# Attention in a fused attention and two-layer MLP kernel: full-row transposes of q and k, and another order of the steps of a pair

## The reference

```python
def _attn_ref(q, k, v, tau):            # q, k, v: 4 x 8 x 576 x 64
    scores = np.matmul(q, k.transpose(0, 1, 3, 2)) / np.sqrt(64)
    thresh = np.max(scores, axis=-1, keepdims=True) - tau
    scores = np.where(scores >= thresh, scores, -1e9)
    attn = np.exp(scores - np.max(scores, axis=-1, keepdims=True))
    attn = attn / (np.sum(attn, axis=-1, keepdims=True) + 1e-09)
    return np.matmul(attn, v)
# heads are put side by side: x is 2304 x 512
h = x @ w_in1; g = s * relu(h)**2 + b; x = g @ w_out1     # 512 -> 2048 -> 512
h = x @ w_in2; g = relu(h) + alpha * min(h, 0); out = g @ w_out2
```

## Time and profile before

| what | value |
|---|---|
| median of 3 runs | 1110.75 us (1110.47 to 1111.75) |
| the profiled execution | 1110.12 us, its span 1108.3 us |
| mean granted TensorE clock | 0.995 |
| busy: PE, DVE, ACT, POOL | 1095.1, 525.2, 509.3, 257.9 us |

### The profile page before, as it was taken

How to read it: one execution, slowest core, us unless ns; L and a number is a source line. 1 busy time by engine, 2 the same in 40 slices (tenths; PEclk the granted TensorE clock), 3 DMA queues, 4 the chain that set the end, 5 groups by cost and what they waited for, 6 DMA issues and landing times.

```text
span 1108.3 us, 18964 instructions
## 1 busy us (share of the span) xinstructions
PE 1095.1 (99%) x5826; PEld 892.5 (81%) x5826; DVE 525.2 (47%) x1014; ACT 509.3 (46%) x946; POOL 257.9 (23%) x438
## 2 busy tenths in 40 slices
PE   7999999999999999999999999999999999999998
PEld 6777777777678888888888889888888888888897
DVE  5988888898633242242242236522322332332232
ACT  3878778787744332232232234544433333333343
POOL 2656666565564300000000004422000000000000
PEclk8999999999999999999999999999999999999999
DMA  8666565665111100000000003211100000010010
GB/s 194 144 148 155 136 154 141 148 148 129 44 51 48 54 1 1 1 0 0 0 0 0 0 8 89 86 48 38 39 0 0 30 8 0 0 38 0 0 39 20
DMA packets 86554, 59.28 MB, mean 53 GB/s; under 512 B 49376, under 2 KB 69872, under 8 KB 86512
## 3 DMA queue, kind: packets, MB, share of 16 engines
q1 hardware_dynamic: 82048, 57.28, 20.2%
q10 hardware_dynamic: 4464, 1.48, 0.6%
HBM read 30.94 MB, written 4.72 MB: 32 GB/s over the span
## 4 chain that ended last, share of the span: by engine, by line
PE 94%; DVE 3%; ACT 1%; issue 1%; DMA 0%; POOL 0%; ACTq 0%; POOLq 0%; DVEq 0%
PE psum L934 23%; PE psum L936 23%; PE psum L935 23%; PE psum L1068 6%; PE psum L1034 5%; PE psum L963 3%; PE psum L965 3%; PE psum L1063 2%; DVE act_r L870 2%; PE psum L944 2%; PE psum L1042 1%; ACT win_hi L589 1%; PE psum L1031 1%; PE psum L1073 1%; ACT act_r L704 0%
## 5 line engine op out<-in xcount | busy, mean ns | idle before, releaser
L936 PE MATMUL psum<-x_hi,win_lo 128*128 128x512 f32 (+1 forms) x640 | 238.7, 373 | 0.0
L934 PE MATMUL psum<-x_hi,win_hi 128*128 128x512 f32 (+1 forms) x640 | 238.2, 372 | 0.0
L935 PE MATMUL psum<-x_lo,win_hi 128*128 128x512 f32 (+1 forms) x640 | 238.2, 372 | 0.0
L935 PEld LDWEIGHTS psum<-x_lo,win_hi 128*128 128x128 f32 x640 | 120.2, 188 | 24.0
L934 PEld LDWEIGHTS psum<-x_hi,win_hi 128*128 128x128 f32 x640 | 120.3, 188 | 23.0
L936 PEld LDWEIGHTS psum<-x_hi,win_lo 128*128 128x128 f32 x640 | 120.2, 188 | 23.0
L881 DVE SCALAR_TENSOR_TENSOR act_r<-act_n,nalpha,act_r 128x512 f32<-128x512 f32 (+1 forms) x80 | 56.2, 702 | 160.1 <-ACT act_r L715 159.8
L870 DVE SCALAR_TENSOR_TENSOR act_r<-act_r,s_c 128x512 f32<-128x512 f32 (+1 forms) x80 | 72.4, 905 | 116.4 <-ACT act_r L704 116.4
L612 ACT ACTIVATE ex<-psum,negm 128x576 f32<-128x576 f32 x144 | 107.6, 747 | 39.9 <-DVE negm L786 38.8
L707 ACT ACTIVATE g_hi<-act_r,b_c 128x512 fp32r<-128x512 f32 (+1 forms) x80 | 54.5, 682 | 152.5 <-PE psum L936 122.4
L546 POOL TENSOR_SCALAR ex<-ex,none_in,rinv 128x576 f32<-128x576 f32 x142 | 117.5, 827 | 19.8 <-DVE rinv L805 13.4
(11 more groups left out here) (97 smaller groups left out, 1622.4 us busy)
## 6 DMA issues: line engine op xcount, KB each, us to landing
k_twice<-k_hi SPq DMA_DIRECT2D x64, 144.0 KB, 2.5
stage<-in_moe_w_out_dram SPq DMA_DIRECT2D x32, 256.0 KB, 2.5
out_dram<-stage SPq DMA_DIRECT2D x18, 256.0 KB, 2.2
q_both<-q_hi SPq DMA_DIRECT2D x32, 128.0 KB, 2.3
q_both<-q_lo SPq DMA_DIRECT2D x32, 128.0 KB, 2.3
win_raw<-in_moe_w_in_dram SPq DMA_DIRECT2D x16, 256.0 KB, 2.9
stage<-in_moe_w_in_dram SPq DMA_DIRECT2D x16, 256.0 KB, 2.6
raw_q<-in_q_dram SPq DMA_DIRECT2D x30, 128.0 KB, 2.4
```

The source lines that it names most:

```text
L934: nc.tensor.matmul(dst, lhs[0], rhs[0], start=first, stop=False)
L935: nc.tensor.matmul(dst, lhs[0], rhs[1], start=False, stop=False)
L936: return nc.tensor.matmul(dst, lhs[1], rhs[0], start=False, stop=final)
```

## The change

It does these things:

- `fill_qk` transposes the last 64 rows of q and k as full transposes of 128 rows; the rows 64 to 127 of that part of `raw_q` and `raw_k` are set to zero once by DVE. q takes five transposes of 128x128, k six.
- raw_k of pair 1 is loaded by SyncE, behind q of pair 1, and no longer by ACT.
- In `LAYOUT`, K moves from place 3 to place 5, tiles 2 and 3 to places 3 and 4.
- In `TURNS`, T0 moves from step 8 to 4, T1 to 8, T2 to 9, the first tails to 10, T6 to 12, the second tails to 13.
- The first group with v moves from step 16 to 15.
- ACT copies the first group's o at step 16 and the second's at 20, each in front of the exp of that step. `copy_last` and the loads of the opening go in front of the copies of transposed tiles.
- The banks of the hand-written end of the last pair follow from the new order.

```diff
-        LAYOUT = ["Q", 0, 1, "K", 2, 3, "L", 4, 5, 6, 7, 8]
+        LAYOUT = ["Q", 0, 1, 2, 3, "K", "L", 4, 5, 6, 7, 8]
-        TURNS = [(8, 0, False), (9, 1, False), (10, 2, False), (10, 3, False), (11, 0, True),
-                 (11, 4, False), (12, 5, False), (13, 6, False), (13, 7, False), (14, 4, True)]
+        TURNS = [(4, 0, False), (8, 1, False), (9, 2, False), (10, 3, False), (10, 0, True),
+                 (11, 4, False), (12, 5, False), (12, 6, False), (13, 7, False), (13, 4, True)]
-        PV = {16: [(0, 0), (0, 1), (0, 2), (0, 3), (0, 4)], 20: [(1, 0), (1, 1), (1, 2), (1, 3), (1, 4)],
+        PV = {15: [(0, 0), (0, 1), (0, 2), (0, 3), (0, 4)], 20: [(1, 0), (1, 1), (1, 2), (1, 3), (1, 4)],
-        PADDED = 5
+        PADDED = 7
-        FIRST_OUT, SECOND_OUT = 20, 20
+        FIRST_OUT, SECOND_OUT = 16, 20
-                    self.bank = [shared[0], psum[:, 4, :], psum[:, 5, :], shared[0]][LATE.index(number)]
+                    self.bank = [late_bank, psum[:, 4, :], psum[:, 5, :], late_bank][LATE.index(number)]
-            return shared[1] if static(n) and n == FINAL else shared_bank("o", group)
+            return other_bank if static(n) and n == FINAL else shared_bank("o", group)
+        late_bank = shared_bank("turn", LATE[0])
+        other_bank = shared[1 - RUNS.index((0, "turn", LATE[0])) % 2]
             load_raw_q(sp, 1, 1)
+            load_raw_k(sp, 1, 1)
...
                 t, after, later = Use(n0, l), Use(n0, l + 1), Use(n0, l + 2)
-                if after.tile:
-                    exp(after)
                 for group, at in ((0, FIRST_OUT), (1, SECOND_OUT)):
                     out_of = Use(n0, l - at)
                     if out_of.pos == 0 and out_of.inside:
                         o_copy(out_of.pair, group)
+                if after.tile:
+                    exp(after)
+                if later.turns_last:
+                    copy_last(later)
+                if static(n0) and n0 == 0:
+                    opening_loads(l)
                 for turn in turns_at(n0, l):
                     copy_turned(turn)
                 if later.prepares:
                     qk_high(later)
-                if later.turns_last:
-                    copy_last(later)
-                if static(n0) and n0 == 0:
-                    opening_loads(l)
...
-                if l == K1_AT:
-                    load_raw_k(act, 1, 1)
...
+            for raw in (raw_q, raw_k):
+                nc.vector.memset(raw[LAST:P, :, QT - 1, :], 0.0).then_inc(padded, 1)
...
-                last = raw[0:LAST, t.prep_parity, QT - 1, :]
-                for c in range(QT - 1):
-                    nc.tensor.transpose(dst[:, first + c * P:first + (c + 1) * P], raw[:, t.prep_parity, c, :], ident[:])
+                chunks = [(first + c * P, c) for c in range(QT)]
                 if t.prep:
-                    nc.tensor.transpose(dst[:, first - LAST:first], last, ident[0:LAST, 0:LAST])
-                end = first + (QT - 1) * P
-                nc.tensor.transpose(dst[:, end:end + LAST], last, ident[0:LAST, 0:LAST]).then_inc(filled, 1)
+                    chunks = [(first - LAST, QT - 1)] + chunks
+                for col, c in chunks:
+                    mm = nc.tensor.transpose(dst[:, col:col + P], raw[:, t.prep_parity, c, :], ident[:])
+                mm.then_inc(filled, 1)
```

More of the change, by code:

```diff
@@ L679, in opening_loads @@
                     load_raw_v(act, 1, 1, [V1_AT.index(l)])
-            K1_AT, V0_AT, Q2_AT, V1_AT = -2, [0, 1, 2], 3, [5, 6, 7]
+            V0_AT, Q2_AT, V1_AT = [0, 1, 2], 3, [5, 6, 7]
             load_raw_k(act, 0, 0)
```

## The result

| | before | after | forecast |
|---|---|---|---|
| median | 1111.38 us (1110.47 to 1113.43, 8 runs) | 1115.13 us (1114.42 to 1116.03, 8 runs) | 1115.8 |
| the profiled execution | 1110.12 us | 1115.20 us | 1115.2 |
| interval of tile 7's maximum, 12 in the loop, mean | 17.63 us | 18.29 us | 18.28 |
| last interval | 17.58 us | 17.09 us | 17.11 |
| tile 7's maximum of pair 0 | 27.17 us | 22.35 us | near 23.1 |

The ratio is 1.0031, its 95% interval 1.0022 to 1.0039: slower by 0.3%.

The account below looks back on a forecast made before the run. DVE and POOL were taken to bound each interval up to tile 7's transposes, PE the rest. Intervals +8.5, opening -3.0, tail -0.45 sum to +5.0 on 1110.12; with 0.63 for the median, 1115.8 us, range 1109.5 to 1120.

Parts of the forecast that it names:

- P to T7: From the second P V group's start to tile 7's first transposes: set by DVE and POOL, stays 10.71 us.
- T7 to P: From tile 7's transposes to the next pair's second P V group: PE work with one stall, 6.91 us before.
- (1): Full-row transposes of q and k: save PE 0.44 us a pair, hidden before tile 7's transposes, priced at 0.
- (2): Work moved past tile 7's transposes: t2 leaves (-0.53), k (+0.65) and T0 (+0.43) come, t6's stall goes (-0.28).
- (3): Score tile t5 waits for k_lo to free k's PSUM bank: 0.39 us a pair, bounds 0 and 0.7.
- (4): ACT's o copies, the second ahead of t6's exp: 0, with no slack; 0.1 us a pair if ACT is slower.
- (5): Opening: the wait for raw_k goes, part is lost to k_twice's landing: -3.0 us, bounds 0 and -4.8.
- (6): Tail: T0 out of the way shortens PE's 0.63 us wait for ACT: -0.45 us, bounds 0 and -0.6.
- A: Rival: PE's time is the bound wherever it is spent, so faster, about 1100 us; chance 0.13.
- B: Rival: k's split does not stall t5, so no change, 1110.3 us, interval near 17.9; chance 0.19.
- C: Rival: opening gives nothing, first P V group waits for T7's copy, 0.1 us a pair: 1120 us; chance 0.10.
- D: Rival: the drain comes also with full rows, k carries 0.20 us more past T7: 1118.6 us; chance 0.03.

Follow-up runs that it names:

- experiment 1: The kernel before with only the full-row transposes of q and k and the two memsets they need: 1111.66 us, ratio 0.9994.
- 11: The changed kernel with three of q's transposes issued twice, 0.33 us more TensorE work a pair: 1115.81 us, ratio 1.0036 to the kernel before.
- 12: The changed kernel with three of k's transposes issued twice, 0.33 us more TensorE work a pair: 1119.48 us, ratio 1.0066 to the kernel before.
- experiment 7: The changed kernel with the old 64-row transposes again: 1115.82 us, ratio 1.0040 to the kernel before.
- Experiment 2: The changed kernel with the first P V group back at step 16, so k goes ahead of it: 1113.68 us, ratio 1.0014 to the kernel before.
- 9: The kernel before with full-row transposes, raw_k of pair 1 by SyncE, and POOL's none_in of t8 one step later: 1107.22 us, ratio 0.9954.
- 10: The kernel before with raw_k of pair 1 by SyncE and POOL's none_in of t8 one step later, without full-row transposes: 1106.71 us, ratio 0.9956.
- Experiment 3: The changed kernel with T0 back at step 8 and T1 at 9: 1116.84 us, ratio 1.0042 to the kernel before.
- experiment 4: The kernel before with raw_k of pair 1 loaded by SyncE alone: 1107.27 us, ratio 0.9958.
- 8: The kernel before with full-row transposes, raw_k of pair 1 by SyncE and DVE's reciprocal ahead of the mask: 1114.94 us, ratio 1.0027.
- experiment 5: The kernel before with full-row transposes and DVE's reciprocal ahead of the mask: 1120.57 us, ratio 1.0060.
- experiment 6: The kernel before with DVE's reciprocal ahead of the mask alone, transposes still over 64 rows: 1120.14 us, ratio 1.0072.

## Why the prediction was right

**What bounds the kernel.** Right. The interval falls into P to T7, which is set by other engines, and T7 to P, which is PE's. Experiments 1 and 11 show the first (0.44 us less and 0.33 us more change nothing), 12 the second. The last pair's interval had said it.

**(1) Full rows at 0.** Right for the kernel before (experiment 1). In the new order k lies behind T7, where the sum charged 0.65 for it; with 64-row transposes it would have cost 0.07 more (experiment 7), not the 0.14 that PE saves.

**(2) and (3) What moves past T7, and t5's stall.** The stretch measured 7.56 us (mean of the loop), the sum had 6.91 + 0.66 = 7.57. That k stands there for t2 is in this length, and was not tested alone. The stall is 0.42 + 0.10 - 0.13 = 0.39 (t5's second start comes 0.24 behind its first, 0.10 over pace), as taken; its links, k_hi 0.70 and k_lo 0.82, are those of the earlier trace rows. Experiment 2 removes it by itself. One sentence on what bounds the kernel was incomplete: the rest of the interval is not only "PE work with one stall". A second chain, to the mask of t1, reaches t3's fill just in time (experiments 9 and 10). The sum did not suffer, as in the new order t3 takes the bank of t0.

**(4) The copies of o at 0.** Not tested alone, but the trace bears it out: the exp of t6, behind the copy, ends at 97.87, and the mask starts at P + 4.41, where it was P + 4.42. ACT's and DVE's timelines:

```profile
97.12 0.75 ACT L616 ACTIVATE ex<-psum,negm 128x576 f32<-128x576 f32 x1
```

```profile
97.90 0.82 DVE L796 SCALAR_TENSOR_TENSOR ex<-psum,thr,ex 128x576 f32<-128x576 f32 x1
```

Experiment 3 shows how little slack ACT has further on: there the exp of t8 starts 0.31 us later behind P, and T7 0.11 later.

**(5) Opening, -3.0.** The maximum of pair 0 came 4.82 us earlier instead of 4.1, and the first interval of 19.94 gave 1.79 back: -3.03. The place was the one named, the landing of `k_twice` (2.23 us). That the sum came out is partly luck: the maximum was 0.7 us earlier than forecast, and 1.79 were lost again where 0.5 to 1.7 were allowed and 1.1 taken. The clock was full throughout, which the step had left open; what it gave and what the load gave was not taken apart.

**(6) Tail, -0.45.** Measured -0.42, but not where the step put it. The wait ahead of the first tails fell from 0.63 to 0.24 us, yet the block behind them now waits 0.85, where it followed at once:

```profile
299.32 0.44 PE L1035 MATMUL psum<-ident,ex 128*128 128x128 f32 x2 [0.24 <-ACT pt L638]
300.61 1.09 PE L1038 MATMUL psum<-ident,ex 128*128 128x128 f32 x8 [0.85 <-ACT pt L638]
```

The kernel before had one block more there, four transposes at 293.82, in PE's timeline:

```profile
293.82 0.66 PE L1034 MATMUL psum<-ident,ex 128*128 128x128 f32 x4 [0.24 <-ACT pt L634]
...
295.60 1.13 PE L1034 MATMUL psum<-ident,ex 128*128 128x128 f32 x8
```

Counted from the maximum of pair 15, the tails now start where those four did (2.31 us), and the block of eight where the tails did (3.60). What is gone is the stretch from the tails to the block of eight, 295.60 - 295.11 = 0.49 us; 0.07 is lost again behind it. So T0's place shortened the tail, as the step said, but by one block less in the line and not by a shorter wait: the waits there grew, from 1.07 us to 1.33 with the one at 301.94. The figure was right by luck.

**The sum.** The intervals gave 12 x 0.66 + 2 x 0.53 - 0.49 = +8.5, as forecast (the first is set at the 18.15 of the forecast here, and what it has above that is counted in the opening); with the opening and the tail that is the +5.08 us of 1115.20 - 1110.12, against +5.0. Between medians it is 3.75 us, since the profiled execution of before was one of its quicker ones: of the 48 executions of the kernel before, 28 had the mean clock of the traces with 17.1 us at the low clock (0.992), and these were the slower ones (experiment 4); the profiled one was not of them. The forecast had no term for how the executions of one kernel differ.

**The rivals.** A and B fell: 18.29 is neither 17.2 nor 17.9. C's wait of the first P V group for T7's copy did not appear. D fell: six transposes of k start 0.66 us before L, 0.109 each. Of the signs named, one was off: T6 waited 0.34 us for POOL, not half a microsecond.

## What to carry to other kernels

Split a period where the bound changes hands, and price an edit by the side it lands on: here the same 0.33 us of TensorE cost 0.01 or 0.34. Work moved to the uncovered side makes a kernel slower even while the engine gets less to do. Before shortening a chain, look for the one that ends just behind it; and test the parts of a bundle apart, for one of them (k of pair 1 by SyncE) alone made the kernel 0.4% faster.

## What the runs showed of the hardware

- The length of the low clock (1.2 GHz) in the opening differs with small edits, 17.1 us in the trace of experiment 1, 10.2 in that of the kernel before, 6.8 in that of 4, 3.4 in that of 8, none in the changed kernel's; and, by the mean clock, between executions of one kernel. It goes with 1.6 us between the two groups of the kernel before (experiment 4), and with 5.4 us between the executions of experiment 5 at 0.992 and the single one at 1.000. The Trainium skill (TensorE: Matmul & The Clock Gate, Part 1: The HAM clock gate) says that how much runs at the low clock varies from run to run of one kernel, and the mean clocks agree.
- One DVE operation on 128x2, den, took 0.63 us instead of 0.16 while POOL normalised (experiment 6), and ended with it. In all the traces together, the 144 times that den on 128x2 started 0.2 us or more into a normalisation it ended with it and took 0.27 to 0.63 us; the 168 times that it started within 0.05 us of one's start it took 0.17; den on 128x1 took 0.14 although it started 0.19 to 0.53 us into one (161 times). The Trainium skill (SBUF — State Buffer, Who interferes with whom) tells of a port pair of the two that, for DVE's 2-port modes, the one that issues first holds for a whole instruction. The rows fit that; that den runs in such a mode none of them shows.
